# A gated layer: the low halves of all five normalised value tiles on VectorE

## What is computed

```python
h = x @ w_in
h = 0.5 * h * (1.0 + np.tanh(c * (h + 0.044715 * h ** 3)))
u, v = (h[..., :d_ff // 2], h[..., d_ff // 2:])
mu = np.mean(v, axis=-1, keepdims=True)
var = np.mean((v - mu) ** 2, axis=-1, keepdims=True)
v_n = (v - mu) / np.sqrt(var + 1e-06) * g_ln
v_s = np.einsum('ts,bsd->btd', w_sg, v_n) + b_sg[None, :, None]
gated = u * v_s
return (x + gated @ w_out).astype(np.float32)
```

## Time and profile before

| what | value |
|---|---|
| median of 3 runs | 1093.39 us (1088.6, 1093.39, 1094.24) |
| the profiled execution | 1091.62 us |
| its span in the profile | 1089.8 us |
| TensorE busy | 1017.6 us, 93% |
| VectorE busy | 603.0 us, 55% |
| ScalarE busy | 459.9 us, 42% |
| GpSimd busy | 392.5 us, 36% |
| gated layer in the trace | about 460 to 715 us |

### The profile page before, as it was taken

How to read it: one execution, slowest core, us unless ns; L and a number is a source line. 1 busy time by engine, 2 the same in 40 slices (tenths; PEclk the granted TensorE clock), 3 DMA queues, 4 the chain that set the end, 5 groups by cost and what they waited for, 6 DMA issues and landing times.

```text
span 1089.8 us, 25230 instructions
## 1 busy us (share of the span) xinstructions
PE 1017.6 (93%) x9616; PEld 879.7 (81%) x9616; DVE 603.0 (55%) x1209; ACT 459.9 (42%) x898; POOL 392.5 (36%) x310
## 2 busy tenths in 40 slices
PE   3999999999999999898989899899999999999998
PEld 2766666666666666578889797888899999999998
DVE  3677777777777777588474847445322222212221
ACT  2577777777777776533231413133112111201210
POOL 3776666666666665431010203268000000000000
PEclk9999999999999999989999899899999999999999
DMA  6344344434343333300000000133000000000000
GB/s 217 89 111 109 108 112 113 111 108 108 108 108 108 109 88 98 116 25 1 1 0 0 0 0 1 52 87 115 1 1 22 22 22 0 22 22 0 22 22 22
DMA packets 34015, 64.80 MB, mean 59 GB/s; under 512 B 4160, under 2 KB 17088, under 8 KB 33984
## 3 DMA queue, kind: packets, MB, share of 16 engines
q1 hardware_dynamic: 33984, 64.37, 20.6%
HBM read 41.81 MB, written 4.72 MB: 43 GB/s over the span
## 4 chain that ended last, share of the span: by engine, by line
PE 65%; issue 22%; DVE 5%; ACT 3%; POOL 3%; DMA 1%; SPq 0%; ACTq 0%; DVEq 0%; POOLq 0%
PE ps L662 12%; PE ps L696 12%; PE ps L698 12%; PE ps L697 11%; PE ps L645 9%; PE ps L604 5%; DVE prob L1064 2%; POOL n_l L564 2%; ACT prob L888 2%; PE ps L633 1%; PE ps L634 1%; PE ps L635 1%; DVE pT L1079 1%; ACT xT L879 1%; DMA stage<-in_moe_w_in 1%
## 5 line engine op out<-in xcount | busy, mean ns | idle before, releaser
L1064 DVE TENSOR_SCALAR_CACHE_REDUCE prob<-ps 128x1152 f32<-128x1152 f32 x144 | 195.5, 1358 | 96.4 <-PE ps L645 76.2
L507 POOL TENSOR_SCALAR prob<-prob,rsum 128x1152 f32<-128x1152 f32 x144 | 176.7, 1227 | 138.8 <-DVE rsum L1073 138.2
L888 ACT ACTIVATE prob<-prob,nmax 128x1152 f32<-128x1152 f32 x144 | 181.4, 1259 | 20.9 <-DVE prob L1064 13.3
L662 PE MATMUL ps<-pT,v_sb 128*64 128x288 f32 x1152 | 171.7, 420 | 14.6 <-ACT xT L879 12.2
L879 ACT ACTIVATE pT<-ps 128x512 f32<-128x512 f32 (+1 forms) x288 | 110.2, 435 | 116.1 <-PE ps L604 115.8
L645 PE MATMUL ps<-k_over,q_over 64*128 64x288 f32 x768 | 141.2, 318 | 2.3 <-DVE prob L1064 2.3
L1027 ACT ACTIVATE f_h<-ps 128x288 fp32r<-128x288 f32 x96 | 39.4, 410 | 245.8 <-PE ps L698 245.8
L645 PEld LDWEIGHTS ps<-k_over,q_over 64*128 64x128 f32 x768 | 110.5, 193 | 22.7 <-DVE prob L1064 21.6
L662 PEld LDWEIGHTS ps<-pT,v_sb 128*64 128x64 f32 x1152 | 71.8, 137 | 56.7 <-issue 19.1
L604 PEld LDWEIGHTS ps<-ident,prob 64*128 64x128 f32 x2592 | 101.7, 142 | 17.8 <-issue 17.8
L696 PE MATMUL ps<-f_h,c_h 128*128 128x288 f32 x384 | 113.7, 296 | 0.0
(11 more groups left out here) (128 smaller groups left out, 2376.3 us busy)
## 6 DMA issues: line engine op xcount, KB each, us to landing
q_raw<-in_q SPq DMA_DIRECT2D x16, 640.0 KB, 5.1
k_raw<-in_k SPq DMA_DIRECT2D x16, 576.0 KB, 3.9
v_sb<-in_v SPq DMA_DIRECT2D x32, 288.0 KB, 2.9
k_over<-kh SPq DMA_DIRECT2D x32, 144.0 KB, 2.5
k_over<-kl SPq DMA_DIRECT2D x32, 144.0 KB, 2.6
out_x<-yT SPq DMA_DIRECT2D x8, 576.0 KB, 3.1
q_over<-qh SPq DMA_DIRECT2D x32, 128.0 KB, 2.2
q_over<-ql SPq DMA_DIRECT2D x32, 128.0 KB, 2.3
```

What stands on the lines that cost most here:

```text
L507: g.tensor_scalar(sl, sl, rsum[:, s:s + 1], 0.0, ALU.mult, ALU.add).then_inc(norm_done, 1)
L662: ins = te.matmul(ps[PH * c:PH * c + PH, ACC_BANK, 0:n], v_sb[:, a, j, :], pT[:, a, j, c * n:c * n + n], start=(j == 0), stop=(j == KB - 1))
L888: sc.activation(sl, sl, ACT.Exp, scale=-1.0, bias=nmax[:, s:s + 1], accum_out=esum[:, s:s + 1]).then_inc(exp_done, 1)
L1064: ve.tensor_scalar(prob[:, PROB_BUF[s], :].rearrange("p (c n) -> p c n", c=SCORE_BANKS), ps[:, 0:SCORE_BANKS, 0:CK], -SCALE, BIG, ALU.mult ...
```

## The change

`norm_lo` moves from GpSimd's block to VectorE's and takes over `tail_lo`. VectorE now calls it for each v tile m at the end of the step in which that tile was normalised: after the `gelu` of the next element. All five low halves count one semaphore, `n_ready`, five a batch; `n_stacked` is gone, and the waits of TensorE and of `gelu` are rewritten to it. GpSimd keeps `norm_rstd` alone. The subtraction itself, its operands and where the result lies are the same.

```diff
-            def norm_lo(b, m):
-                pool.wait_ge(n_hi, at(b, TT, m + 1))
-                pool.nop(nofuse=True)
-                g.tensor_tensor(n_l[:, m, :], v_f[:, m % 3, :], n_h[:, m, :].bitcast(F32),
-                                ALU.subtract).then_inc(n_ready, 1)
-
             with pool.Fori(0, B) as b:
-                norm_rstd(b, 0)
-                for m in range(1, TT):
+                for m in range(TT):
                     norm_rstd(b, m)
-                    norm_lo(b, m - 1)
...
                         if e == 4 and c == 0:
-                            if m < TT - 1:
-                                pe.wait_ge(n_ready, at(b, TT - 1, m + 1))
-                            else:
-                                pe.wait_ge(n_stacked, at(b, 1, 1))
+                            pe.wait_ge(n_ready, at(b, TT, m + 1))
...
                 if n >= 3:
-                    dve.wait_ge(n_ready, at(b, TT - 1, n - 2))
+                    dve.wait_ge(n_ready, at(b, TT, n - 2))
...
-            def tail_lo(b):
-
-                dve.wait_ge(n_hi, at(b, TT, TT))
-                ve.tensor_tensor(n_h[QL:P, TT - 1, :], v_f[0:QL, (TT - 1) % 3, :],
-                                 n_h[0:QL, TT - 1, :].bitcast(F32), ALU.subtract).then_inc(n_stacked, 1)
+            def norm_lo(b, m):
+
+                dve.wait_ge(n_hi, at(b, TT, m + 1))
+                r = rows(m)
+                lo = n_l[:, m, :] if m < TT - 1 else n_h[QL:P, m, :]
+                ve.tensor_tensor(lo, v_f[0:r, m % 3, :], n_h[0:r, m, :].bitcast(F32), ALU.subtract)\
+                    .then_inc(n_ready, 1)
...
                     gelu(b, e - 1, chain)
-                    if e == V_AT[TT - 1] + 3:
-                        tail_lo(b)
+                    if GELU[e - 2][0] == "v":
+                        norm_lo(b, GELU[e - 2][1])
                 gelu(b, GT - 1, chain)
```

More of the change, by code:

```diff
@@ L240, in build @@
         n_ready = sem("n_ready")
-        n_stacked = sem("n_stacked")
         gate_ready = sem("gate_ready")
```

## The result

| | before | after |
|---|---|---|
| median of 4 runs | 1093.7 us (1088.6 to 1094.24) | 1067.2 us (1065.23 to 1067.53) |
| ratio | | 0.977, 95% interval 0.975 to 0.979 |
| span of the profiled execution | 1089.8 us | 1065.5 us |
| last attention copy into `xT` to last residual add of the gated layer | 459.3 to 714.0: 254.7 us | 457.1 to 689.7: 232.6 us |

The change made the kernel 2.3% faster; the forecast was 1070 us, range 1065 to 1077. By it the layer became 22.1 us shorter. The rest of the 24.3 us between the two spans is attention, which ended 2.2 us earlier in the second profile; behind the layer both took 375.8 us.

What follows compares the result with a forecast made beforehand. TensorE was taken as the bound, busy 1017.6 of 1089.8 us, with stalls behind VectorE's late chain. Stalls 16.9 plus clock 6.3 less 0.3 gave 22.9 us off, so 1068.7 or 1070.5, forecast 1070, range 1065 to 1077.

Steps and rivals of the forecast that it cites:

- The normalise at 0.54 without GpSimd beside it: VectorE's `v_f` normalise of tiles 1 to 4 falls from 1.50 to 0.54 us each, 3.84 us off the chain.
- A low half on VectorE at 0.69: Each new 128x512 subtract on VectorE takes about 0.69 us, 0.61 net of overlap, 2.44 us for four.
- The collision with `rstd`: Rival: VectorE's low halves stand still beside GpSimd's `rstd`, 0.57 us each, 8.4 us in all, giving 1079; chance 0.06.
- The tail at 555.79: Second batch: tail's low half starts on VectorE at 555.79 instead of 559.82, leaving 0.19 us slack before TensorE needs it.
- The shares of the chain: VectorE's changes before the tail's low half: -3.84 normalise, +2.44 low halves, -0.41 and -0.24 waits, -1.98 forward move.
- The last batch, 0.3 us: Tail's low half meets GpSimd's `t_h` splitting `w_tok1`, costing TensorE about 0.3 us, or 2.7 if `t_l` follows directly.
- The clock: Slow matmuls behind the tail's stall in three batches vanish, gaining 6.3 us; rival that it falls anyway: 1077, chance 0.03.
- its sign of a clock at 1.00 to the end of the layer: Sign of being right: granted clock 1.00 in every 5 us from 475 us to the gated layer's end.
- The sum, 22.9 us: Gain over all batches: 16.9 us of TensorE stalls plus 6.3 of clock, less 0.3 in the last batch.
- 1.84 in the sum: TensorE's waits at pair 3 for VectorE's GELU of tile 4, all four batches: 1.84 us gained.
- 14.14 + 0.96 + 6.3 - 0.3: TensorE's tail stall 14.14, wait for `n_l` of tile 3 0.96, clock 6.3, less 0.3 for the last batch's collision.
- The whole time: Forecast 1070 us for the kernel: 1068.7 from the profiled 1091.62, 1070.5 from the median 1093.39.

Runs made afterwards that it cites:

- e3: Changed kernel plus an unneeded GpSimd 128x512 subtract on a spare tile where GpSimd's low halves stood, behind rstd of the next tile; 1080.14 us.
- e4: Kernel before, GpSimd order only: low half of tile m directly behind rstd of tile m, ahead of rstd of tile m + 1; 1073.31 us.
- e9: Changed kernel plus unneeded GpSimd subtracts on a spare tile, each directly behind rstd of its own tile; 1067.42 us.
- e2: Kernel before with only the tail's low half moved forward, behind u1's multiply; GpSimd keeps the other four; 1080.88 us.
- e0: The changed kernel itself run again, beside the kernel before on the same chip; 1068.16 us.
- e12: The changed kernel run once more, for comparison with other kernels on the same chip; 1065.75 us.
- e10: Kernel before, with GpSimd's low half directly behind rstd of its own tile and VectorE's tail low half behind u1's multiply; 1066.57 us.
- e11: Kernel before with GpSimd's low halves reordered, tail forward, last-batch terms of pairs 8 and 9 regrouped, and w_tok1 splitting started one pair later; 1063.93 us.
- e5: Changed kernel with VectorE making each of the four 128-row low halves twice, once into a spare tile; 1080.16 us.
- e1: Changed kernel with the tail's low half put back where it stood, behind u3's poly and u2's multiply; 1078.3 us.

## Why the prediction was right, step by step

- **The normalise at 0.54 without GpSimd beside it:** measured 541 ns median; e3 brings the slow one back, e4 and e9 show the place. Shown.
- **A low half on VectorE at 0.69:** 682 ns. Shown.
- **The collision with `rstd`:** it exists, the other way round. `rstd` now takes 0.93 us where a low half stands beside it, 0.55 where none does, and the normalise behind it starts on time; VectorE's instruction had started first (534.63 against 534.79). It costs nothing, as was argued. The rule of the Trainium skill, "SBUF — State Buffer", section "Who interferes with whom", that a VectorE instruction with two SBUF inputs contends with a GpSimd instruction that reads SBUF, agrees with this trace (0.93 against 0.55). GpSimd's timeline, against the earlier trace rows:

```profile
534.79 0.93 POOL L557 TENSOR_TENSOR rstd<-var_e,minus_half 128x1 f32<-128x1 f32 x1 [15.97 <-DVE var_e L1142]
540.31 0.55 POOL L557 TENSOR_TENSOR rstd<-var_e,minus_half 128x1 f32<-128x1 f32 x1 [4.60 <-DVE var_e L1142]
```

- **The tail at 555.79:** 555.49; slack 0.34 where 0.19 was worked out. The shares of the chain held: the move alone is 1.98 us in e2.
- **The last batch, 0.3 us:** 0.29. The low half met `t_h` and took 1308 ns; GpSimd's second instruction, `t_l`, did not get in ahead of it.
- **The clock:** the falls behind the tail's stalls went with the stalls (three of three). What was not foreseen is one fall behind the gates' stalls of 1.58 and 0.17 us in the last batch: 12 matmuls 0.24 us apart. The prediction reckoned with no stall at all, though this one stands in the trace of before at 701.32, and its sign of a clock at 1.00 to the end of the layer failed here. The fall came in some executions of the changed kernel and not in others (in `after` and e0, not in e12). It is 1.6 of the 2.4 us between layers of 232.6 and 230.2 (211.9 against 210.4 from the first normalise on, before rounding 1.56); the rest is the fall at the layer's start.
- **The sum, 22.9 us:** from the first normalise to the last residual add the kernel before took 234.4 us, `after` 211.9 and e12 210.4. That is 22.4 us with the fall behind the gates and 24.0 without it, so the waits and falls that the prediction summed were worth 1.1 us more than the sum. By the starts of the same matmuls in before and e12, the stretches of pairs 1 to 3 shrank by 2.2 us in all (1.84 in the sum), and those of pairs 4 to 7 by 21.8 (14.14 + 0.96 + 6.3 - 0.3 = 21.1 in the sum).
- **The whole time:** the median fell by 26.5 us, 3.6 more than the sum (24.5 and 26.3 beside e0 and e12). The pair of profiles accounts for 24.3 of it: 22.1 in the layer and 2.2 of attention, which is scatter. The rest is that the profiled execution of before, 1091.62 us, was 2.1 us faster than its median, and that of `after` was at its median. So that the forecast of 1070 came within 3 us of 1067.2 is in part luck: the unforeseen fall cost 1.6 us and hid the 1.1 us that the waits gave beyond the sum, and the scatter is of the same size. Why executions of the same kernel differ is only in part known. The profiled execution of before has a mean granted clock of 0.987; nine other executions of it, sorted by time, with their clocks:

```
1089.82 0.986   1090.37 0.987   1091.75 0.984   1092.12 0.983   1092.63 0.984
1093.65 0.983   1094.45 0.984   1094.45 0.984   1095.47 0.980
```

  Where the clock is lower the time tends to be longer. With 6.3 us for three falls a fourth, behind the stall of the first batch, would by this estimate be worth about 2 more. That the slower executions have it is not shown: no profile of one exists, and a fall can stand elsewhere too. e0_after has one in attention (0.68 in 430 to 435 us), e4, e10 and e11 have one at about 35 to 45 us.

## What to carry to other kernels

When an instruction of one engine takes different times on one shape, look at what GpSimd ran at that moment before costing any change; then try the order on GpSimd first, since e4 got 19 of about 25 us by moving nothing between engines. Cost a stall of TensorE together with the slow matmuls behind it, and take the time of "before" from many executions, because falls of the clock come and go. Compare profiles over the stretch that the change can reach, since a fall ahead of it differs from execution to execution. When one stall is filled, count the matmuls up to the wait, not up to the end of the filler.

## What the runs showed of the hardware

TensorE's clock fell behind some stalls and not behind others of the same length. Idle time shown at the tail, all kernels: 1.00, 1.39, 1.47, 1.49 and 1.55 us, fourteen stalls, no fall; 1.77, one, a fall; 2.57, two, one fall; 2.97, a fall; 2.98 and 2.99, three, two falls; 3.38, 3.85 and 4.56, three falls. The pair of 1.58 and 0.17 us in the last batch had a fall in five profiles (after, e0, e2, e3, e5) and none in six (before, e1, e4, e9, e10, e12). What decides between equal stalls was not settled.

VectorE's normalise (one SBUF input) and its subtract (two) each stood still until GpSimd's instruction had ended: the normalise ended 0.28 us behind it, the subtract 0.54 us (`after`, behind `t_h`). The waiting shows as a longer instruction, not as idle time. And GpSimd's `rstd` and spare subtract stood still behind a VectorE subtract that had started first: 0.93 for 0.55, 1.41 for 1.04. In these cases the one that started first ran at its own speed. A waiting normalise did not get in between two GpSimd instructions that followed each other directly: in the last batch of before it stood from 676.81 through `n_l` and through `t_h`, which started at 678.01, and took 2.51 us. VectorE's multiplies and statistics beside the same GpSimd instructions, with one input in PSUM or one input in all, showed no delay (e4: 0.68 and 0.69 us beside an `n_l` of 1.30).
